# State products of a linear-attention kernel: one product of 64 value columns for each head instead of two of 32

## The chip, the cores and the metric

The kernel runs on one core of a Trainium2 chip. The metric is the device time of one execution in microseconds (us). A core has a matrix engine (TensorE, "PE" in the profile, its weight loads "PEld"), three elementwise engines (VectorE "DVE", ScalarE "ACT", GpSimd "POOL") and a queue that starts DMAs (SyncE "SP"). They run their own instruction lists in order and meet at semaphores.

## The reference, cut to what matters

Three stages follow one another: a linear attention with a decaying state, a dense layer pair (384 to 2048 and back, with an ELU between), and a routed layer pair with 8 experts. The change touches the first. It has 2 batches, 8 heads, 768 tokens and 48 features per head:

```python
for t in range(S):
    cur = np.einsum('bhd,bhe->bhde', u[None] * kt, vt)
    y[:, :, t] = np.einsum('bhd,bhde->bhe', rt, state + cur)
    state = w[None, :, :, None] * state + np.einsum('bhd,bhe->bhde', kt, vt)
...
x = moe(x)     # 1536 x 384 -> 2048 -> 384
return moe2(x) # 8 experts, 384 -> 1024 -> 384, capacity 384
```

## The kernel before

The 1536 tokens are cut into 12 chunks of 128, six for each batch. A chunk `c` costs TensorE three pieces of work: `scores(c)` (keys times queries), `outer(c)` (the sum over the chunk's tokens of key times value, which is what the chunk adds to the state), and `back(c)` (old state times queries plus masked scores times values, which is the chunk's output). The last chunk of a batch has no successor, so `outer` runs for ten chunks.

`outer(c)` multiplies `nat`, an SBUF tile that holds for each token r, the keys padded to 64 columns for each head, and the values. Keys of one head (128 tokens x 64) are the weights; values are streamed. The eight heads go as four pairs `hp` with `j` 0 and 1: head `j` writes to partitions `64*j` to `64*j+63` of the PSUM bank `u_bank(c)`, so the two heads of a pair use two column halves of the matrix engine, each with all 128 rows. The 48 value columns of a head are taken as `MAIN` = 32 columns and then 32 more that hold the remaining `REM` = 16 and 16 of zeros (`v_cols`). So there are 4 x 2 x 2 = 16 products of 64 weight columns and 32 streamed columns. All operands are float32, and each such product shows in the trace as two weight loads and two matmul records: 32 of each for a chunk. After the last, semaphore `s_u` lets DVE form the new state (`state`, L904 and L906), which `back` of the next chunk reads.

All PE work of the first two stages is one list, written out by hand. It starts with `scores(0)`, `scores(1)`, `back(0)`, `outer(0)`, `back(1)`, `outer(1)`. Then a loop runs over 6 blocks `n` of 256 tokens and 16 column tiles `f` of the dense layer. Each step issues `fc1(n, f)` (L1193 to L1195 with `xt` as the moving operand), then whatever attention piece has its slot there (`base_slot`, `step_of`), then `fc2` of three steps before (L1193 to L1195 with `g_hi`, `g_lo`). Between fc1 and fc2, DVE, ACT, DVE, ACT and POOL turn one tile into `g_hi` and `g_lo` (L1027, L726, L1030, L728, L596). fc1 waits for L1030 of two steps before. In block 0, ACT and DVE also split the weights into high and low parts as they arrive (L922 for the first layer, L928 for the second), and fc1 waits for L922 at each second `f`. POOL scales the keys by the decay in place (`natural_k1`, L523) before `outer` reads them, and prepares the rest of each chunk (L541, L547, L511, L518, L552) between its L596 steps. DVE's L886 waits for POOL's L518. Chunks 6, 8 and 10 have `outer` right behind `scores`.

Of the kernel before, what the change touches and what calls it, by code (L numbers as in the profile page):

```python
# [12 lines left out]
def build(nc, B, H, S, D, DFF, NE, FE, CAP, rkt_in, nat_in, decay, bonus, win, wout, wgate, wexp, out, slots):  # L13
    T = B * S
    C = 128
    HP = H // 2
# [20 lines left out]
    MAIN = 32  # L37
    REM = D - MAIN
    RN, KN, VM = 0, DM, DM + 64 * H
    VR = VM + MAIN * H  # L40
    NAT = VR + 3 * REM * HP
    WCH = 4
    NWC = FT // WCH
    WCOL = WCH * KT * 128
# [21 lines left out]
    def put(name, shape, dtype, at=None):  # L66

        size = int(np.prod(shape[1:])) * 4
        if at is None:
            at = top[0]  # L70
            top[0] = at + -(-size // 32) * 32
        return nc.alloc_sbuf_tensor_at(name, shape, dtype, offset=at), at + -(-size // 32) * 32

    def new(name, shape, dtype=F32):
        return put(name, shape, dtype)[0]
# [55 lines left out]

    top[0] = a_at
    rkt = [new(f"rkt{p}", [128, 2, HP, C]) for p in range(2)]
    nat = [new(f"nat{p}", [128, NAT]) for p in range(2)]
    r1 = [new(f"r1_{p}", [128, HP, C]) for p in range(2)]
    k1 = [new(f"k1_{p}", [128, HP, C]) for p in range(2)]
    att = [new(f"att_{p}", [128, 2, HP, C]) for p in range(2)]
# [17 lines left out]
    with ctx:  # L155
# [13 lines left out]
        def pair(name):  # L169
            return [sem(f"{name}{p}") for p in range(2)]  # L170
# [15 lines left out]
        s_nat = pair("nat_loaded")  # L186
# [106 lines left out]
        def chunk_at(n, f, k):  # L293

            for c in range(2, NSTEP):
                if base_slot(c) + k == FT * n + f:
                    return c
            return None
# [5 lines left out]
        def is_at(n, f, what, after=0):  # L304

            for c in range(2, NSTEP):
                if base_slot(c) + step_of(c)[what] + after == FT * n + f:
                    return c
            return None
# [9 lines left out]
        def u_bank(c):  # L319
            return ps_x2[c][:, 0:2 * C] if c < 2 else ps_u  # L320
# [19 lines left out]
        def wait_if(eng, s, count):  # L340

            if not (isinstance(count, int) and count <= 0):
                eng.wait_ge(s, count)
# [20 lines left out]
        def _(sp):  # L364
# [5 lines left out]
            def load_nat(c):  # L370
                wait_if(sp, s_rku, c - 1)
                wait_if(sp, s_y, c - 1)
                if c in (2, 3):
                    sp.wait_ge(s_u, c - 1)
                sp.dma_start(nat[c % 2][:, :], nat_in[c, :, :]).then_inc(s_nat[c % 2], 16)

            def load_nat_rk(c):
                sp.dma_start(nat[c][:, 0:VM], nat_in[c, :, 0:VM]).then_inc(s_nrk[c], 16)
# [1 line left out]
            def load_nat_v(c):  # L380
                sp.dma_start(nat[c][:, VM:NAT], nat_in[c, :, VM:NAT]).then_inc(s_nat[c], 16)

# [25 lines left out]
            load_rkt(2)  # L408
            load_out(0)
            load_nat(2)  # L410
            load_in(2)
            load_in(3)
            load_out(1)
            load_rkt(3)
            load_out(2)
            load_nat(3)
            load_out(3)
            sp.dma_start(gate_w[:, :, :], wgate).then_inc(s_gw, 16)
            sp.wait_ge(s_const, NPOOLC)
            for c in range(4, NSTEP):  # L420
                load_rkt(c)
                load_nat(c)
                if c - 4 < NBLANK // 2:
                    blank_rows(c - 4)
# [763 lines left out]
        def _(pe):  # L1188
            mm = nc.tensor.matmul

            def product(dst, w_hi, w_lo, x_hi, x_lo, start, stop):

                mm(dst, w_hi, x_hi, start=start, stop=False)  # L1193
                mm(dst, w_hi, x_lo, start=False, stop=False)  # L1194
                return mm(dst, w_lo, x_hi, start=False, stop=stop)  # L1195
# [17 lines left out]

            def v_cols(c, hp, j):

                h = 2 * hp + j
                main = VM + MAIN * h
                rem = VR + 3 * REM * hp + REM * j
                return nat[c % 2][:, main:main + MAIN], nat[c % 2][:, rem:rem + MAIN]

            def outer(c):

                pe.wait_ge(s_k1n, c + 1)
                if c < 2:
                    pe.wait_ge(s_nat[c], 16)
                else:
                    pe.wait_ge(s_xhi, 2 * c)
                    pe.wait_ge(s_xlo, 2 * c)
                for hp in range(HP):
                    for part in range(2):  # L1230
                        for j in range(2):
                            key_cols = slice(KN + 128 * hp + 64 * j, KN + 128 * hp + 64 * j + 64)
                            at = 64 * hp + MAIN * part
                            last = mm(u_bank(c)[64 * j:64 * j + 64, at:at + MAIN], nat[c % 2][:, key_cols],  # L1234
                                      v_cols(c, hp, j)[part], start=True, stop=True, skip_group_check=True)
                last.then_inc(s_u, 1)

            def back(c):
# [28 lines left out]
                for j in range(2):  # L1267
                    for hp in range(HP):
                        mm(dst(2 * j, hp), v_cols(c, hp, j)[0], att[p][:, j, hp, :], start=not old, stop=True,
                           skip_group_check=True)  # L1270
                for j in range(2):
                    for hp in range(HP):
                        last = mm(dst(1, hp), v_cols(c, hp, j)[1], att[p][:, j, hp, :], start=False, stop=j == 1,
                                  skip_group_check=True)
# [7 lines left out]
            for hp in range(HP):  # L1282
                last = nc.tensor.transpose(ps_y[1][:, 128 * hp:128 * hp + 128], pwk2[:, hp, :], ident[:, :])
# [4 lines left out]
            scores(1)  # L1288
            back(0)
            outer(0)  # L1290
            back(1)
            outer(1)

            def fc1(n, f):
# [69 lines left out]
            for n in range(NB):  # L1364
                for f in range(FT):
                    fc1(n, f)
                    c = chunk_at(n, f, 0)
                    if c is not None:
                        scores(c)
                    c = is_at(n, f, OUTER)  # L1370
                    if c is not None and leaves_state(c):
                        outer(c)
                    c = is_at(n, f, BACK)
                    if c is not None:
                        back(c)
                    if n and f == F_T:
                        for t in range(BT):
                            x2_transpose(n - 1, t)
                    if n and f == F_LG:
                        logits(n - 1)  # L1380
                    if n and f == F_CNT:
                        count(n - 1)
                    if n == NB - 1 and f == F_A:
                        early_x()
                    if f >= LAG:
                        fc2(n, f - LAG)
                    elif n:
                        fc2(n - 1, FT + f - LAG)
# [16 lines left out]
            def tile_fc2(f):  # L1405
                g = slice(f * C, (f + 1) * C)
                cols = slice(W1 + f * DM, W1 + (f + 1) * DM)
                return product(ps_y[0][:, 0:DM], ge_hi_tile[:, g], ge_lo_tile[:, g], we_hi[:, cols],
                               we_lo[:, cols], f == 0, f == ET - 1)
# [26 lines left out]
            for f in range(ET // 2, ET):  # L1436
                last = tile_fc2(f)
# [79 lines left out]
            for kt in range(KT):  # L1517
                last = nc.tensor.transpose(ps_xt[0][:, 128 * kt:128 * kt + 128], xrow[0][:, 1, 128 * kt:128 * kt + 128],
                                           ident[:, :])
# [7 lines left out]
            for kt in range(KT):  # L1527
                last = mm(ps_e[0][:, :], xe_lo[0][:, kt, C:SN], we_hi[:, kt * FE:kt * FE + HALF], start=False,
                          stop=kt == KT - 1)
# [7 lines left out]
            for f in range(ET):  # L1537
                if f % (ET // 2) == 0:
                    pe.wait_ge(s_gelo, ET // 2 + f)
                last = tile_fc2(f)  # L1540
# [9 lines left out]
            with pe.If(over > SN):  # L1550
                with pe.Fori(0, NOVER) as e:
                    pe.wait_ge(s_dld, 32 * (e + 1))
                    for kt in range(KT):
                        last = nc.tensor.transpose(ps_xt[0][:, 128 * kt:128 * kt + 128],
                                                   xrow[0][:, 0, 128 * kt:128 * kt + 128], ident[:, :])
# [3 lines left out]
                    for f in range(ET):  # L1559
                        for kt in range(KT):  # L1560
                            cols = slice(kt * FE + f * 128, kt * FE + (f + 1) * 128)
                            last = product(ps_e[f % 2][:, 0:128], we_hi[:, cols], we_lo[:, cols],
                                           xe_hi[0][:, kt, 0:128], xe_lo[0][:, kt, 0:128], kt == 0, kt == KT - 1)
# [3 lines left out]
                        last = product(ps_ye[0][:, 0:DM], ge_hi[:, f % 4, 0:128], ge_lo[:, f % 4, 0:128],  # L1567
                                       we_hi[:, cols], we_lo[:, cols], f == 0, f == ET - 1)
# [73 lines left out]
```

## Time and profile before

| | |
|---|---|
| Time, median of 3 runs | 444.85 us (444.45 to 445.5) |
| Profiled execution, its own time | 444.44 us |
| Its span, first to last instruction | 442.7 us |
| PE busy | 424.6 us (96%) |
| DVE, ACT, POOL busy | 246.0, 183.3, 232.2 us |
| Mean granted TensorE clock | 0.996 |
| Attention and dense layers | from 0 to about 284 us |
| Routed layers | from about 284 us to the end |

Busy time is the union of an engine's instructions, and a matmul's recorded duration covers more than the time for which it holds the engine. So what a group of products costs is read from its first start to the start of what comes next on PE, not from its durations.

### The profile page before, as it was taken

To read this page: it belongs to the slowest core of one execution; us is meant where nothing else is said; L and a number is where in the kernel's file an instruction comes from. 1 tells how busy PE (TensorE), PEld (TensorE's weight loads), DVE (VectorE), ACT (ScalarE), POOL (GpSimd) and SP (SyncE) were. 2 spreads that over 40 slices of the span, in tenths; PEclk is the share of its full clock that TensorE was granted. 3 is DMA by queue.
4 is the path that set the end of the run, shared out by engine and by line. 5 is a ranking of instruction groups with operands and counts; after the bars stand their busy time and mean duration, and the time that the engine had idled before them with its cause. 6 is when DMAs were issued, how large, how long until landed. Compare 5 with 4: busy or idle time off the path is not lost.

```text
span 442.7 us, 9569 instructions
## 1 busy us (share of the span) xinstructions
PE 424.6 (96%) x3764; PEld 406.0 (92%) x3764; DVE 246.0 (56%) x595; ACT 183.3 (41%) x390; POOL 232.2 (52%) x240
## 2 busy tenths in 40 slices
PE   8789999999999999999999999989999999999994
PEld 7679999999999999899999999876999999999994
DVE  7978763665366536744564477553355454553521
ACT  4256542333332323243333445333454564465520
POOL 1888775549554955396534334114434726628431
PEclk9999999999999999999999999989999999999999
DMA  7993977113200311020008000720837548357100
GB/s 248 391 402 114 377 243 281 56 40 108 80 33 23 125 48 66 3 99 2 1 14 327 0 1 36 286 89 13 291 91 304 207 147 339 131 215 299 54 31 26
DMA packets 16826, 62.40 MB, mean 141 GB/s; under 512 B 2043, under 2 KB 9509, under 8 KB 14736
## 3 DMA queue, kind: packets, MB, share of 16 engines
q1 hardware_dynamic: 14992, 57.08, 35.8%
q0 software_dynamic: 1792, 4.73, 2.8%
q8 instruction: 29, 0.48, 0.4%
q14 instruction: 13, 0.11, 0.1%
HBM read 49.38 MB, written 13.21 MB: 141 GB/s over the span
## 4 chain that ended last, share of the span: by engine, by line
PE 70%; POOL 11%; issue 7%; DVE 7%; DMA 2%; ACT 2%; SPq 0%; POOLq 0%; DVEq 0%; ACTq 0%
PE bank L1193 20%; PE bank L1195 19%; PE bank L1194 19%; POOL g_lo L596 3%; DMA rkt<-rkt 2%; PE bank L1351 2%; PE bank L1234 1%; POOL slots L574 1%; POOL nat L523 1%; ACT elu L726 1%; DVE elu L1027 1%; PE bank L1338 1%; POOL rku L511 1%; DVE elu L1030 1%; POOL rku L518 1%
## 5 line engine op out<-in xcount | busy, mean ns | idle before, releaser
L596 POOL TENSOR_TENSOR g_lo<-elu,g_hi 128x256 fp32r<-128x256 f32 x95 | 74.7, 786 | 102.6 <-ACT g_hi L728 101.3
L726 ACT ACTIVATE elu<-elu 128x256 f32<-128x256 f32 x96 | 40.2, 418 | 111.3 <-DVE elu L1027 111.2
L1193 PE MATMUL bank<-xt,wd_hi 128*128 128x256 f32 x288 | 81.6, 284 | 2.5 <-DVE wd_lo L922 1.2
L1195 PE MATMUL bank<-xt,wd_lo 128*128 128x256 f32 x288 | 81.1, 281 | 0.0
L1194 PE MATMUL bank<-xt,wd_hi 128*128 128x256 f32 x288 | 81.0, 281 | 0.0
L1027 DVE TENSOR_SCALAR elu<-bank 128x256 f32<-128x256 f32 x96 | 40.3, 420 | 49.9 <-PE bank L1195 49.6
L1193 PE MATMUL bank<-wd_hi,g_hi 128*128 128x384 f32 x192 | 67.4, 351 | 0.0
L1030 DVE SCALAR_TENSOR_TENSOR elu<-elu,bank 128x256 f32<-128x256 f32 x96 | 40.4, 421 | 47.9 <-ACT elu L726 47.4
L1194 PE MATMUL bank<-wd_lo,g_hi 128*128 128x384 f32 x192 | 64.5, 336 | 0.0
L1195 PE MATMUL bank<-wd_hi,g_lo 128*128 128x384 f32 x192 | 64.4, 336 | 0.0
L728 ACT CAST g_hi<-elu 128x256 fp32r<-128x256 f32 x96 | 39.0, 406 | 46.8 <-DVE elu L1030 45.8
L1193 PEld LDWEIGHTS bank<-xt,wd_hi 128*128 128x128 f32 x288 | 54.1, 188 | 4.2 <-DVE elu L1030 2.2
L1195 PEld LDWEIGHTS bank<-xt,wd_lo 128*128 128x128 f32 x288 | 54.5, 189 | 0.0
L1194 PEld LDWEIGHTS bank<-xt,wd_hi 128*128 128x128 f32 x288 | 54.3, 189 | 0.0
L1128 DVE SCALAR_TENSOR_TENSOR ge_lo<-bank,ge_hi 128x256 fp32r<-128x256 f32 x56 | 23.8, 425 | 49.2 <-ACT ge_hi L783 49.2
L611 POOL TENSOR_TENSOR wd_lo<-wd_raw,wd_hi 128x1024 fp32r<-128x1024 f32 x12 | 28.5, 2396 | 37.2 <-ACT wd_hi L796 24.2
L783 ACT ACTIVATE ge_hi<-bank 128x256 fp32r<-128x256 f32 x56 | 21.5, 385 | 54.2 <-PE bank L1195 26.9
L1193 PEld LDWEIGHTS bank<-wd_hi,g_hi 128*128 128x128 f32 x192 | 36.4, 189 | 1.7 <-issue 1.0
L1194 PEld LDWEIGHTS bank<-wd_lo,g_hi 128*128 128x128 f32 x192 | 36.4, 190 | 0.0
L1195 PEld LDWEIGHTS bank<-wd_hi,g_lo 128*128 128x128 f32 x192 | 36.0, 188 | 0.0
L611 POOL TENSOR_TENSOR we_lo<-we_raw,we_hi 128x1024 fp32r<-128x1024 f32 x9 | 21.3, 2398 | 26.9 <-ACT we_hi L796 26.9
L1193 PE MATMUL bank<-we_hi,ge_hi 128*128 128x384 f32 x64 | 22.5, 351 | 2.2 <-DVE ge_lo L1083 2.2
(199 smaller groups left out, 964.3 us busy)
## 6 DMA issues: line engine op xcount, KB each, us to landing
we_raw<-wexp SPq DMA_DIRECT2D x8, 1536.0 KB, 7.5
wd_raw<-wexp SPq DMA_DIRECT2D x8, 1536.0 KB, 7.6
nat<-nat SPq DMA_DIRECT2D x10, 672.0 KB, 4.3
rkt<-rkt SPq DMA_DIRECT2D x12, 512.0 KB, 6.5
xrow<-slots SPq DMA_DIRECT2D x16, 193.0 KB, 7.1
wd_raw<-win SPq DMA_DIRECT2D x4, 768.0 KB, 8.7
wd_raw<-wout SPq DMA_DIRECT2D x4, 768.0 KB, 10.5
slots<-blank SPq DMA_DIRECT2D x1, 2702.0 KB, 14.0
```

What stands on the lines that cost most here:

```text
L596: nc.gpsimd.tensor_tensor(g_lo[:, f % 4, :], elu[:, f % 2, :], g_hi[:, f % 4, :].bitcast(F32), ALU.subtract).then_inc(s_glo, 1)
L611: nc.gpsimd.tensor_tensor(EL[r][:, cols], ER[r][:, cols], EH[r][:, cols].bitcast(F32), ALU.subtract).then_inc(s_elo2[r], 1)
L726: nc.scalar.activation(elu[:, f % 2, :], elu[:, f % 2, :], ACT.Exp).then_inc(s_exp, 1)
L728: nc.scalar.copy(g_hi[:, f % 4, :], elu[:, f % 2, :]).then_inc(s_ghi, 1)
L783: nc.scalar.activation(ge_hi[:, f % 4, :], ps_e[f % 2][:, 0:SN], ACT.Relu).then_inc(s_gehi, 1)
L1027: V.tensor_scalar_min(elu[:, f % 2, :], ps_h[f % 2][:, 0:BN], 0.0).then_inc(s_m, 1)
L1030: V.scalar_tensor_tensor(out=elu[:, f % 2, :], in0=elu[:, f % 2, :], scalar=-1.0, in1=ps_h[f % 2][:, 0:BN], op0=ALU.add, op1=ALU.max).then ...
L1128: V.scalar_tensor_tensor(out=ge_lo[:, f % 4, :], in0=ps_e[f % 2][:, 0:SN], scalar=0.0, in1=ge_hi[:, f % 4, :].bitcast(F32), op0=ALU.max, o ...
L1193: mm(dst, w_hi, x_hi, start=start, stop=False)
L1194: mm(dst, w_hi, x_lo, start=False, stop=False)
L1195: return mm(dst, w_lo, x_hi, start=False, stop=stop)
L1351: last = mm(ps_lg[:, NE * t:NE * (t + 1)], x2t[:, t, 128 * kt:128 * kt + 128], gate_w[:, kt, :], start=kt == 0, stop=kt == KT - 1)
```

## The change

The values of a pair of heads are laid out differently in `nat`: main columns of head 1, main columns of head 0, remainder of head 0, 16 zeros, remainder of head 1 (112 columns for a pair, as many as before). Head 0's 64 columns then lie in one run, and head 1's are two runs of 32 whose starts lie 80 columns apart. `outer` streams them as one moving operand of 2 x 32 columns, written to the same 64 PSUM columns as before. Its 16 products of 32 columns become 8 of 64. The SBUF tile `nat` is 48 columns wider (the second run's view reaches past the data), so tiles behind it move by 192 or 384 bytes; the bytes that a DMA brings are the same. `back` takes its two 32-column pieces from their new places. The host lays out the input.

```diff
-    VR = VM + MAIN * H
-    NAT = VR + 3 * REM * HP
+    VP = 2 * MAIN + 3 * REM
+    NAT = VM + VP * HP
...
-    nat = [new(f"nat{p}", [128, NAT]) for p in range(2)]
+    nat = [new(f"nat{p}", [128, NAT + 3 * REM]) for p in range(2)]
...
-                h = 2 * hp + j
-                main = VM + MAIN * h
-                rem = VR + 3 * REM * hp + REM * j
+                main = VM + VP * hp + MAIN * (1 - j)
+                rem = VM + VP * hp + 2 * MAIN + REM * j
                 return nat[c % 2][:, main:main + MAIN], nat[c % 2][:, rem:rem + MAIN]
+
+            def v_both(c, hp, j):
+
+                step = MAIN + 3 * REM if j else MAIN
+                main = VM + VP * hp + MAIN * (1 - j)
+                return nat[c % 2][:, main:main + 2 * step].rearrange("s (k n) -> s k n", k=2)[:, :, 0:MAIN]
...
                 for hp in range(HP):
-                    for part in range(2):
-                        for j in range(2):
-                            key_cols = slice(KN + 128 * hp + 64 * j, KN + 128 * hp + 64 * j + 64)
-                            at = 64 * hp + MAIN * part
-                            last = mm(u_bank(c)[64 * j:64 * j + 64, at:at + MAIN], nat[c % 2][:, key_cols],
-                                      v_cols(c, hp, j)[part], start=True, stop=True, skip_group_check=True)
+                    for j in range(2):
+                        key_cols = slice(KN + 128 * hp + 64 * j, KN + 128 * hp + 64 * j + 64)
+                        last = mm(u_bank(c)[64 * j:64 * j + 64, 64 * hp:64 * hp + 64].rearrange("p (k n) -> p k n", k=2),
+                                  nat[c % 2][:, key_cols], v_both(c, hp, j), start=True, stop=True,
+                                  skip_group_check=True)
                 last.then_inc(s_u, 1)
```

Nothing changes places in any engine's list. On PE, the rows from `back(0)` to the first fc1 stood like this before (numbers behind `x` count equal rows; 64x32 is partitions and columns of the result):

```order
 L1269 MATMUL bank<-att_104,nat_98 32x128 x8
 L1273 MATMUL bank<-att_104,nat_98 32x128 x8
 L1234 MATMUL bank<-nat_98 64x32 x16
 L1262 MATMUL bank<-r_1_101,z_110 32x128 x8
 L1265 MATMUL bank<-r_1_101,z_110 32x128 x4
```

and stand like this now (L1234 is L1237, and the lines of `back` are four higher):

```order
 L1273 MATMUL bank<-att_104,nat_98 32x128 x8
 L1277 MATMUL bank<-att_104,nat_98 32x128 x8
 L1237 MATMUL bank<-nat_98 64x64 x8
 L1266 MATMUL bank<-r_1_101,z_110 32x128 x8
 L1269 MATMUL bank<-r_1_101,z_110 32x128 x4
```

The other nine places read alike: 16 products of 32 columns became 8 of 64. DVE, ACT, POOL and SP have the same lists as before.

## Rows read from the trace of the kernel before

**Rows 1.** The page: busy time, and shares of the chain that ended last.

```profile
PE 424.6 (96%) x3764; PEld 406.0 (92%) x3764; DVE 246.0 (56%) x595; ACT 183.3 (41%) x390; POOL 232.2 (52%) x240
...
PE 70%; POOL 11%; issue 7%; DVE 7%; DMA 2%; ACT 2%; SPq 0%; POOLq 0%; DVEq 0%; ACTq 0%
```

**Rows 2.** L1234 alone by stretch: length, PE and PEld busy (count), clock, DMA.

```profile
0.00:29.20 29.20, 2.44 (x64) 2.11 (x64) 1.00 0.90 338
29.20:53.10 23.90, 2.25 (x64) 2.03 (x64) 1.00 0.74 258
53.10:245.00 191.90, 6.75 (x192) 6.08 (x192) 1.00 0.27 94
```

**Rows 3.** PE in order, 63.9 to 68.5 us: start, length, engine, work.

```profile
63.92 1.16 PE L1209 MATMUL bank<-r,k 64*128 64x128 f32 x16
65.01 0.44 PE L1193 MATMUL bank<-wd_hi,g_hi 128*128 128x384 f32 x1
...
67.34 1.12 PE L1234 MATMUL bank<-nat 128*64 128x32 f32 x32
68.40 0.44 PE L1193 MATMUL bank<-wd_hi,g_hi 128*128 128x384 f32 x1
```

**Rows 4.** PE in windows of 0.02 to 0.3 us: same columns, length to the last end.

```profile
67.34 0.25 PE L1234 MATMUL bank<-nat 128*64 128x32 f32 x2
...
67.34 0.31 PE L1234 MATMUL bank<-nat 128*64 128x32 f32 x4
...
67.34 0.37 PE L1234 MATMUL bank<-nat 128*64 128x32 f32 x6
...
63.92 0.49 PE L1209 MATMUL bank<-r,k 64*128 64x128 f32 x4
...
63.92 0.83 PE L1209 MATMUL bank<-r,k 64*128 64x128 f32 x10
```

**Rows 5.** PE in order, part of `back` of one chunk, 73.4 to 74.4 us.

```profile
73.44 0.62 PE L1269 MATMUL bank<-att,nat 128*32 128x128 f32 x16
73.87 0.62 PE L1273 MATMUL bank<-att,nat 128*32 128x128 f32 x16
```

**Rows 6.** POOL, DVE, PE in order, 17 to 30 us; [idle before <-what ended it].

```profile
17.10 1.28 POOL L541 TENSOR_TENSOR k<-rkt,pwk 128x512 f32<-128x512 f32 x1 [1.11 <-issue]
...
23.68 0.55 DVE L886 TENSOR_REDUCE bon<-rku 128x8 f32<-128x384 f32 x1 [0.48 <-POOL rku L518]
...
27.60 1.50 DVE L922 TENSOR_TENSOR wd_lo<-wd_raw,wd_hi 128x768 fp32r<-128x768 f32 x1
...
29.24 0.36 PE L1193 MATMUL bank<-xt,wd_hi 128*128 128x256 f32 x1 [1.24 <-DVE wd_lo L922]
```

**Rows 7.** DVE and PE, 33 to 54 us; last, DVE's waits for PE, 24 to 59.

```profile
33.60 0.95 DVE L922 TENSOR_TENSOR wd_lo<-wd_raw,wd_hi 128x768 fp32r<-128x768 f32 x1
...
51.70 0.95 DVE L928 TENSOR_TENSOR wd_lo<-wd_raw,wd_hi 128x768 fp32r<-128x768 f32 x1
53.09 0.42 DVE L1027 TENSOR_SCALAR elu<-bank 128x256 f32<-128x256 f32 x1 [0.44 <-PE bank L1195]
...
34.79 0.28 PE L1193 MATMUL bank<-xt,wd_hi 128*128 128x256 f32 x1
...
DVE elu L1027 <- PE bank L1195: 0.4, 1, 0.4
```

**Rows 8.** PEld's waits, 100 to 200 us (total, times, longest), then POOL, DVE in order.

```profile
PEld bank L1234 <- POOL nat L523: 0.7, 3, 0.2
...
107.93 1.27 POOL L523 TENSOR_TENSOR nat<-nat,pwn 128x512 f32<-128x512 f32 x1
...
112.74 0.42 DVE L1027 TENSOR_SCALAR elu<-bank 128x256 f32<-128x256 f32 x1 [2.61 <-PE bank L1195]
...
135.69 0.43 DVE L1027 TENSOR_SCALAR elu<-bank 128x256 f32<-128x256 f32 x1 [0.94 <-PE bank L1195]
```

**Rows 9.** All engines, 270 to 300 us; the number behind POOL's count is the clock.

```profile
270.00:300.00 30.00, 27.73 (x158) 24.56 (x157) 18.27 (x49) 12.85 (x24) 7.65 (x9) 0.94 0.41 152
```

More of the change, by code:

```diff
@@ L374, in load_nat @@
                     sp.wait_ge(s_u, c - 1)
-                sp.dma_start(nat[c % 2][:, :], nat_in[c, :, :]).then_inc(s_nat[c % 2], 16)
+                sp.dma_start(nat[c % 2][:, 0:NAT], nat_in[c, :, :]).then_inc(s_nat[c % 2], 16)
             def load_nat_rk(c):
@@ L1599, in natural @@
         k_pad[:, :, :, :D] = k
-        rem = np.zeros((n, c, HP, 3, REM), np.float32)
-        rem[:, :, :, 0] = v[:, :, 0::2, MAIN:]
-        rem[:, :, :, 2] = v[:, :, 1::2, MAIN:]
-        return np.concatenate([r.reshape(n, c, -1), k_pad.reshape(n, c, -1), v[:, :, :, :MAIN].reshape(n, c, -1),
-                               rem.reshape(n, c, -1)], axis=2)
+        v_pair = np.zeros((n, c, HP, 2 * MAIN + 3 * REM), np.float32)
+        v_pair[:, :, :, 0:MAIN] = v[:, :, 1::2, :MAIN]
+        v_pair[:, :, :, MAIN:2 * MAIN + REM] = v[:, :, 0::2]
+        v_pair[:, :, :, 2 * MAIN + 2 * REM:] = v[:, :, 1::2, MAIN:]
+        return np.concatenate([r.reshape(n, c, -1), k_pad.reshape(n, c, -1), v_pair.reshape(n, c, -1)], axis=2)
     def per_head(a):
```

## The prediction, made before the changed kernel ran

> **What bounds the kernel now.** I read the page first. PE is busy 96% of the span and holds 70% of the chain that ended last [rows 1], so time taken off PE counts unless PE then waits for something else. The second view is the edited line by stretch [rows 2]: its 320 records are 32 for each of ten chunks, two chunks before 29.2 us, two more up to 53.1, six after. The third is PE in order of time, which tells what one call of `outer` costs: it starts at 67.34 and the next fc2 starts at 68.40, so 1.06 us [rows 3]. Ten of them are 10.6 us, 2.4% of the span. Last come the waits around these places [rows 6 to 8], because the three kinds of place differ.
>
> **What sets the 1.06 us.** The windows that cut into one `outer` show records in pairs, one for each column half. From the second pair to the third the last end moves from 0.31 to 0.37 us, and over the whole group from 0.25 (first pair) to 1.12 (sixteenth): 0.87/15 = 0.058 us a pair [rows 3, 4]. The next work starts 0.06 us before the last recorded end (68.46 against 68.40). Is that pace set by the weight loads (64 columns) or by streaming 32 columns? `scores` has twice the weight columns (128) and four times the streamed ones (128), also two tiles at a time. It moves from 0.49 to 0.83 us over three pairs, 0.11 us each [rows 4], about twice the pace of `outer`, not four times. And `back` streams 128 columns with only 32 weight columns in four tiles: 16 records in 73.87 - 73.44 = 0.43 us, 0.11 us for each record of a tile [rows 5]. So 0.11 is the price of streaming 128 columns, 64 would cost 0.055 and 32 would cost 0.027. `outer` pays 0.058 where its stream needs 0.027: the loads set its pace, one 64-column load for each half in 0.058 us. With 64 streamed columns the stream takes 0.055 and stays under the load.
>
> **The sum for one `outer`.** Removed: 16 of 32 load-and-product records. Added: 32 more columns in each remaining one. After it there are 8 pairs at 0.058. The first pair ends 0.25 us after the start with 32 columns; with 128 it ends at 0.49 - 0.11 = 0.38 [rows 4]; between them for 64 columns, 0.29. The group then takes 0.29 + 7 x 0.058 = 0.70 us to its last end, and the next work starts 0.065 earlier, at 0.63 (the same difference is 0.07 in `scores`, 65.08 against 65.01 [rows 3]). Saved: 1.06 - 0.63 = 0.43 us. Bounds: the best is half of `scores`, 1.09/2 = 0.55, so 0.51 us saved. The worst without overlap of load and stream is 0.29 + 7 x 0.11 - 0.065 = 1.0, so 0.06 saved. A streamed operand in two runs has no row in this trace. If a break costs nothing, the 0.43 stands; if it made each column cost four times as much, a pair would take 0.22, the whole 1.77 and the change would lose 0.71. I take 0.43, because it is nearest to both measured paces.
>
> A rule speaks against this. The Trainium skill, "TensorE: Matmul & The Clock Gate", section "What overlaps and what doesn't", says that a weight load overlaps running products only where its row group differs; both halves here use all 128 rows. By it load and stream add up: 0.11 us a pair after the change, and nothing is won. But it would also make the pair before 0.058 + 0.027 = 0.085, and the trace has 0.058; in `back`, whose tiles also span all rows, 32-column loads add nothing to the 0.11 us of the stream. The trace disagrees with the rule, so I use the row and keep the rule as a rival.
>
> **Which of the ten count.**
> The first two, at 15 and 19 us: none. DVE's L886 at 23.68 waits for POOL's L518, and POOL's own list had stood still 1.11 us before L541 at 17.10 for something that PE does not give (the row says issue; I take it for the arrival of `rkt`). From there DVE goes on to L922, which ends at 29.10 and releases PE at 29.24 after 1.24 us of idle time [rows 6]. PE reaching that wait 0.86 us earlier only waits longer. Bound: 0 to 0.86 us.
> The third and fourth, at 30.5 and 49.6: together 0.44. fc1 of tile 6 starts at 34.79, its weights' L922 ends at 33.60 + 0.95 = 34.55; the least distance seen is 29.24 - 29.10 = 0.14. So only 0.24 - 0.14 = 0.10 of the third's 0.43 passes. From 24 to 59 us DVE waits for PE once, 0.44 us at 53.09; its L928 ends at 52.65 [rows 7]. PE would offer 0.10 + 0.43 = 0.53 by then, DVE can use 0.44. `back` of chunk 3 waits for the state that DVE makes behind it. Bound: 0 to 0.86.
> The last six, from 67 to 200 us: 6 x 0.43 = 2.58. Three (109.25 and its two likes) wait for POOL's L523, 0.2 us or so each [rows 8]. That is a wait in front of `outer`, so the saving behind it passes; and the POOL and DVE work that leads to it is itself started by PE: DVE stands idle 2.61 us before 112.74 and 0.94 us before 135.69, each ended by PE's fc1 [rows 8]. All this moves with PE, as 0.94 is more than 0.43.
> Behind 200 us there are no more such products. What follows is started by PE's own progress and moves as a block.
>
> **The rest costs nothing.** The DMA of `nat` brings the same bytes. `back` reads pieces of the same size from other columns. SBUF tiles move by at most 384 bytes; no row shows a price for an address, and I give it none (bounds: 0.1 us either way). The state's PSUM columns stay, so DVE's reads do.
>
> **Sum.** 0 + 0.44 + 2.58 = 3.0 us. The profiled execution took 444.44 us, so 441.4; it lay 0.41 under the median 444.85 of the runs, from which it would be 441.8. I predict 441.6. A measurement here tells some 0.2% (0.9 us) from no change.
>
> **Rivals.**
> Half overlap: load and half of the stream add up, 0.058 + 0.027 = 0.085 a pair, 0.29 + 7 x 0.085 - 0.065 = 0.82, 0.24 saved; (6 + 1) x 0.24 = 1.7, time 442.9. For it: in `outer` the pace is 0.058, a little over the 0.055 which half of `scores` would give, so something small is not hidden. Against it: `back`.
> No overlap, by the rule above: 0.06 x 7 = 0.4 saved, 444.2. Against it: the pace before.
> POOL takes over: L523 in front of `outer` at 109, 154 and 199 us keeps its absolute time. Then only the product behind the last of these waits counts, 0.43 us: 444.2. For it: POOL is what PE waits for there, three times. Against it: POOL's chain starts from waits that PE ends, as above.
> All ten count, if the start is led by PE after all: 10 x 0.43 = 4.3, 440.3. Against it: the 1.24 us of idle PE at 29.24.
> Slower: the streamed operand of head 1 jumps 80 columns in the middle, and a stream in two runs is read at a quarter of the rate. Pace 0.22, 0.71 us lost in each: the eight that PE leads lose 5.7 us, and the first two some of their 1.4 where they eat the wait: 450. It decides from a pair over 0.12 us, where 0.29 + 7 x 0.12 - 0.065 = 1.06. For it: no such operand in this trace. Against it: only one jump in 64 columns, and only in half of the products.
> The clock is a disturbance more than a rival: the granted clock falls to 0.94 over 270 to 300 us, behind an idle PE [rows 9]. That is 0.06 x 30 = 1.8 us at one level of loss; that PE work comes 3 us earlier could move or drop that stretch, so plus or minus 1 us is in my range.
>
> **Chances.** Forecast 0.73 (its own range 440.6 to 442.8), all ten 0.05, half overlap 0.07, no overlap 0.07, POOL 0.04, slower 0.04. Faster by over 0.2%: 0.73 + 0.05 + 0.07, less 0.02 for the clock, 0.83. Within 0.2%: 0.07 + 0.04 + 0.02 = 0.13. Slower: 0.04. The range that leaves out at most two in ten goes from 440.3, all ten, to 443.5, past half overlap.
>
> **What would show it.** In the profile after, an `outer` has 16 records, the next PE work starts 0.63 us after its start, and a pair takes 0.058. PE's idle time before 29.2 us grows by up to 0.86 us, most of it at the wait for L922, which ends at the same time. fc1 of tile 6 waits about 0.3 us for L922. DVE's idle time before its L1027 at about 52.7 is gone. The products behind `scores` of chunks 6, 8 and 10 start 0.87, 1.73 and 2.59 us earlier (0.44 and one, three and five times 0.43), the first of them at 108.4. A pair at 0.085 or more, or a start of PE after the first wait earlier than 28.8, makes my sum wrong at its first or its second step.

## The result, and the profile after

The changed kernel takes 441.21 us (median of 7 runs, 440.71 to 442.81) against 444.41 for the kernel before on the same chip (443.96 to 445.5). The ratio is 0.9935, 95% interval 0.9917 to 0.9953, so 2.9 us less, between 2.1 and 3.7. Its profiled execution took 441.02 us with a span of 439.3. The forecast was 3.0 us, and the time forecast was 441.6.

The edited line in the changed kernel, by stretch as in [rows 2], has half the records (the first row has 32 for two chunks) and 6.86 us of busy time instead of 11.44:

```profile
0.00:29.20 29.20, 1.37 (x32) 1.09 (x32) 1.00 0.89 343
29.20:53.10 23.90, 1.37 (x32) 1.09 (x32) 1.00 0.70 243
53.10:245.00 191.90, 4.11 (x96) 3.28 (x96) 1.00 0.28 95
```

PE in order at chunk 4, as in [rows 3], then windows that end in the first, second and third pair of records, as in [rows 4]:

```profile
67.71 0.69 PE L1237 MATMUL bank<-nat 128*64 128x64 f32 x16
68.33 0.44 PE L1193 MATMUL bank<-wd_hi,g_hi 128*128 128x384 f32 x1
...
67.71 0.28 PE L1237 MATMUL bank<-nat 128*64 128x64 f32 x2
...
67.71 0.34 PE L1237 MATMUL bank<-nat 128*64 128x64 f32 x4
...
67.71 0.39 PE L1237 MATMUL bank<-nat 128*64 128x64 f32 x6
```

One `outer` now holds PE for 68.33 - 67.71 = 0.62 us instead of 1.06. The pace is (0.69 - 0.28)/7 = 0.058 us a pair, that of before with twice the streamed columns. This is the first step of the prediction, and it holds.

The start of the program does not. POOL, DVE and PE in order in the changed kernel, as in [rows 6]:

```profile
17.25 1.93 POOL L541 TENSOR_TENSOR k<-rkt,pwk 128x512 f32<-128x512 f32 x1 [1.10 <-issue]
19.14 0.61 POOL L552 TENSOR_TENSOR zw<-z,w_end 128x256 f32<-128x256 f32 x1
19.72 1.90 POOL L547 TENSOR_TENSOR r<-rkt,pw 128x512 f32<-128x512 f32 x1
22.04 1.01 POOL L511 TENSOR_TENSOR rku<-nat 128x384 f32<-128x384 f32 x1 [0.43 <-DMA nat<-nat]
23.20 1.01 POOL L518 TENSOR_TENSOR rku<-rku,u_nat 128x384 f32<-128x384 f32 x1
...
17.10 0.95 DVE L922 TENSOR_TENSOR wd_lo<-wd_raw,wd_hi 128x768 fp32r<-128x768 f32 x1
...
29.70 0.36 PE L1193 MATMUL bank<-xt,wd_hi 128*128 128x256 f32 x1 [1.24 <-DVE wd_lo L922]
```

fc1 of tile 4 starts at 29.70, 0.46 us later than before, though fc1 of tile 0 starts 0.42 us earlier (19.63 against 20.05). Of the 0.46, 0.15 come from L541, which starts that much later in this execution. L541 takes 1.93 us where it took 1.28 [rows 6]. POOL then waits 0.43 us for chunk 2's `nat`. In the kernel before, the same four instructions behind L541 read:

```profile
18.34 1.33 POOL L552 TENSOR_TENSOR zw<-z,w_end 128x256 f32<-128x256 f32 x1
19.64 1.18 POOL L547 TENSOR_TENSOR r<-rkt,pw 128x512 f32<-128x512 f32 x1
20.79 1.72 POOL L511 TENSOR_TENSOR rku<-nat 128x384 f32<-128x384 f32 x1
22.65 1.00 POOL L518 TENSOR_TENSOR rku<-rku,u_nat 128x384 f32<-128x384 f32 x1
```

DVE and POOL around 54 us, as in [rows 7]:

```profile
52.15 0.95 DVE L928 TENSOR_TENSOR wd_lo<-wd_raw,wd_hi 128x768 fp32r<-128x768 f32 x1
53.10 0.42 DVE L1027 TENSOR_SCALAR elu<-bank 128x256 f32<-128x256 f32 x1
54.01 0.42 DVE L1030 SCALAR_TENSOR_TENSOR elu<-elu,bank 128x256 f32<-128x256 f32 x1 [0.49 <-ACT elu L726]
54.35 1.32 DVE L922 TENSOR_TENSOR wd_lo<-wd_raw,wd_hi 128x768 fp32r<-128x768 f32 x1
...
53.67 1.19 POOL L547 TENSOR_TENSOR r<-rkt,pw 128x512 f32<-128x512 f32 x1
```

DVE's 0.44 us of idle time before L1027 is gone, as forecast. But the L922 behind it now runs beside POOL's L547 and takes 1.32 us instead of the 0.95 that this line takes elsewhere, so the state for `back` of chunk 3 gains almost nothing.

From chunk 4 on each `outer` brings what was forecast. The three waits for POOL's L523 are still there and small (as in [rows 8]), and DVE's L1027 is still released by PE, with 2.18 us of idle time instead of 2.61:

```profile
PEld bank L1237 <- POOL nat L523: 0.8, 3, 0.3
...
112.26 0.42 DVE L1027 TENSOR_SCALAR elu<-bank 128x256 f32<-128x256 f32 x1 [2.18 <-PE bank L1195]
```

The last dense tile's fc1 starts at 274.93 us against 277.11 before, 2.18 earlier. The span is 3.4 us shorter. The other 1.2 is the clock, as the first experiment shows: the view of all engines over 270 to 300 us, as in [rows 9], has the clock granted in full here.

```profile
270.00:300.00 30.00, 27.48 (x157) 23.18 (x155) 18.25 (x52) 11.55 (x23) 6.71 (x8) 1.00 0.41 152
```

### The profile page after: what moved, and what is told of

It is laid out like the page before. It is cut to its first block, busy times and chain, and to the rows that moved or that the text cites. A ratio compares the mean times of both kernels' runs of the same rounds, so it can differ in the third digit from the quotient of the medians.

```text
span 439.3 us, 9249 instructions
## 1 busy us (share of the span) xinstructions
PE 418.8 (95%) x3604; PEld 399.6 (91%) x3604; DVE 244.7 (56%) x595; ACT 183.2 (42%) x390; POOL 232.5 (53%) x240
## 4 chain that ended last, share of the span: by engine, by line
PE 65%; DVE 11%; POOL 9%; issue 8%; ACT 3%; DMA 3%; SPq 0%; POOLq 0%; DVEq 0%; ACTq 0%
PE bank L1193 18%; PE bank L1195 18%; PE bank L1194 17%; POOL g_lo L596 3%; ACT elu L726 2%; DVE elu L1027 2%; PE bank L1355 2%; DVE wd_lo L922 2%; DMA rkt<-rkt 1%; POOL slots L574 1%; DVE wd_lo L928 1%; DMA nat<-nat 1%; DVE elu L1030 1%; PE bank L1342 1%; POOL rku L518 1%
## 5 line engine op out<-in xcount | busy, mean ns | idle before, releaser
L1027 DVE TENSOR_SCALAR elu<-bank 128x256 f32<-128x256 f32 x96 | 40.3, 420 | 47.0 <-PE bank L1195 46.6
L616 POOL DMA_INDIRECT out<-yrow,tok_i x16 | 15.7, 983 | 16.6 <-DVE yrow L1148 12.2
```

Of the source, the lines that this page charges most:

```text
L616: nc.gpsimd.indirect_dma_start(out=out, out_offset=bass.IndirectOffsetOnAxis(ap=tok_i[r][:, t, :], axis=0), in_=yrow[r][:, t, :], in_offse ...
L1027: V.tensor_scalar_min(elu[:, f % 2, :], ps_h[f % 2][:, 0:BN], 0.0).then_inc(s_m, 1)
```

## The experiments

Each ratio is to the kernel before, timed beside it. The changed kernel, timed a second time, has 0.9944 (0.9924 to 0.9963). Since a time can't tell 0.4 us, the profiles are read against POOL's first L541, which starts at 16.85 to 17.64 us by run and which PE does not lead. The table holds what the profiles gave, in us behind L541; `nat` is the landing of the last packet of chunk 2's `nat`, in us of the span.

| kernel | L541 takes | `nat` | L518 | fc1 tile 4 | fc1 tile 18 | fc1 tile 95 |
|---|---|---|---|---|---|---|
| before | 1.28 | 20.72 | 5.55 | 12.14 | 52.44 | 260.01 |
| before, again | 1.28 | 20.83 | 5.55 | 12.15 | 52.46 | 260.07 |
| changed | 1.93 | 21.98 | 5.94 | 12.44 | 52.22 | 257.68 |
| changed, again | 1.93 | 22.39 | 6.09 | 12.60 | 52.41 | 257.90 |
| not first two | 1.28 | 21.11 | 5.55 | 12.14 | 51.92 | 257.35 |
| not chunk 0 | 1.29 | 21.24 | 5.54 | 12.15 | 51.92 | 257.35 |
| chunk 0, `rkt` first | 1.28 | 21.34 | 5.54 | 12.13 | 51.91 | 257.36 |
| each twice | 1.28 | 20.99 | 5.54 | 12.33 | 52.71 | 260.47 |
| 96 columns | 2.08 | 21.98 | 6.17 | 12.67 | 52.60 | 258.82 |
| bonus later | 1.94 | 22.25 | 6.19 | 11.44 | 51.74 | 257.21 |

**The kernel before, again.** No edit.

> The kernel before, once more, for a second profile. Theory (the start is set by POOL and the arrival of tiles, and a run moves it by a tenth or two): fc1 of tile 4 starts at 29.0 to 29.5 us, each outer takes 1.06 us, and the time lies within 0.2% of the kernel before. Rival (the start varies by half a microsecond from run to run anyway): fc1 of tile 4 starts 0.4 us or more away from 29.24. The stretch at half clock near 292 us may be missing here; if so the routed layers end about 1.4 us earlier.

444.17 us, ratio 1.0 (0.9983 to 1.0017). The start repeats to 0.01 us once it is counted from L541. No stretch at a lower clock lay near 292 us here:

```profile
270.00:300.00 30.00, 27.54 (x161) 24.02 (x162) 19.57 (x55) 12.74 (x23) 7.65 (x9) 1.00 0.42 152
```

From fc1 of tile 95 to the first warming product (L1442) the first profile has 298.74 - 277.11 = 21.63 us, this one 20.26, the changed kernel 20.22. So the lower clock cost 1.4 us in one execution, and it comes and goes with one and the same kernel. It is no part of the change.

**Each product twice**, to test whether the load sets the pace:

```diff
                 for hp in range(HP):
-                    for j in range(2):
+                    for _ in range(2):
+                        for j in range(2):
```

> New layout, each product of 64 columns is issued twice (the second writes the same values over the first), so there are 16 products a chunk as before, but of 64 columns. Theory (the weight load sets the pace and the stream of 64 columns hides under it): a pair of records still takes 0.058 us, an outer about 1.08 us, time equal to before within 0.5 us. Rival (load and stream add up, in part or whole): a pair takes 0.085 or 0.11 us, an outer 1.5 to 1.9 us, the ten add 3 to 8 us and the time is 447 or more.

444.58 us, ratio 1.0004 (0.999 to 1.0018). PE in order in this kernel:

```profile
67.39 1.15 PE L1238 MATMUL bank<-nat 128*64 128x64 f32 x32
68.47 0.44 PE L1193 MATMUL bank<-wd_hi,g_hi 128*128 128x384 f32 x1
```

Twice the streamed columns of the kernel before, with as many loads, cost 1.08 us against 1.06. The 32 extra columns of each product are all but free, and partial and full addition of load and stream are out.

A rival stays: a fixed cost of each load and product, whatever the columns. The kernel before has a row that speaks against it, with 128 weight columns and only 8 streamed ones:

```profile
81.50 1.40 PE L1351 MATMUL bank<-gate_w,x2t 128*128 128x8 f32 x12
82.75 0.42 PE L1193 MATMUL bank<-wd_hi,g_hi 128*128 128x384 f32 x1
```

Its 12 records take 82.75 - 81.50 = 1.25 us, 0.10 each, where 64 weight columns take 0.058 in each half. The cost grows with the weight columns, so it is the load that the change saves. No run changed the weight columns of `outer` itself.

**96 columns in three runs**, for the first three pairs of heads:

```diff
-                return nat[...][:, main:main + 2 * step].rearrange("s (k n) -> s k n", k=2)[:, :, 0:MAIN]
+                runs = 3 if hp < HP - 1 else 2
+                return nat[...][:, main:main + runs * step].rearrange("s (k n) -> s k n", k=runs)[:, :, 0:MAIN]
```

> As the changed kernel, but the first three pairs of heads of a chunk stream 96 columns in three runs instead of 64 in two; the last 32 land in columns that the next product overwrites, the fourth pair streams 64. Theory (pace is the larger of load, 0.055, and stream, 0.11/128 a column, and breaks in the stream cost nothing): the middle pairs take 0.080 to 0.085 us, an outer about 0.75 us instead of 0.615, the eight that PE leads cost 1.1 us more than the change, time 1.9 under before. Rival 1 (load and stream add up from here): 0.11 to 0.14 a pair, an outer 0.9 or more, 2.3 us or more over the change. Rival 2 (a break costs): the pace lies above 0.09.

442.18 us, ratio 0.9951 (0.9934 to 0.9968). PE's windows that end in the second, third and fourth pair, then the whole:

```profile
67.72 0.39 PE L1239 MATMUL bank<-nat 128*64 128x96 f32 x4
...
67.72 0.47 PE L1239 MATMUL bank<-nat 128*64 128x96 f32 x6
...
67.72 0.55 PE L1239 MATMUL bank<-nat 128*64 128x96 f32 x8
...
67.72 0.83 PE L1239 MATMUL bank<-nat 128*64 128x96 f32 x16
68.47 0.44 PE L1193 MATMUL bank<-wd_hi,g_hi 128*128 128x384 f32 x1
```

0.08 us a pair, which is 96/128 of 0.11. Past the load's 0.058 the stream sets the pace, at the price per column of an unbroken one. Head 1's streams have two breaks and head 0's have none (its step is 32 columns), and the pair goes at the stream's pace all the same. That removes the "slower" rival. An `outer` takes 0.75.

**Only the first two chunks.** `outer` keeps the form with two products of 32 columns for the others:

```diff
-                    for j in range(2):
+                    for part in range(1 if c < 2 else 2):
+                        for j in range(2):
...
+                            if c < 2:
```

> New layout, but only chunks 0 and 1 use one product of 64 columns; the other eight use two of 32. Theory A (faster outers at the start buy nothing, since POOL and DVE set the start): no gain, fc1 of tile 4 at 29.2. Theory B (they cost something: nat of chunk 2 is then in flight together with more weight transfers, lands later and DVE and POOL get in each other's way): fc1 of tile 4 at 29.5 to 29.8, time 0 to 0.5 us above before. Rival (they lead the start): 0.86 us faster.

443.96 us, ratio 0.9984 (0.9965 to 1.0002). The interval reaches from no change to 1.6 us less, so the time excludes neither the 0 of theory A nor the 0.86 of the rival. Its profile can't tell more: over 14 to 22 us the granted clock was 0.81, so its first outer was late and L541 came first. fc1 of tile 4 came 12.53 us behind L541.

```profile
14.00:22.00 8.00, 6.85 (x139) 5.50 (x138) 5.70 (x11) 2.65 (x6) 6.10 (x6) 0.81 0.90 333
```

**All but the first two** (the same edit with `c >= 2`).

> New layout, chunks 0 and 1 use two products of 32, all others one of 64. Theory A: as fast as the full change, 3.0 us under before. Theory B (the first two cost about 0.4 us in the full change): fc1 of tile 4 at 29.2 and fc1 of tile 33 about 1.0 us earlier than before instead of 0.48; time 0.4 us under the full change. Rival: 0.86 us slower than the full change, 2.1 under before.

441.13 us, ratio 0.9925 (0.9907 to 0.9943). The start is back to 12.14, and fc1 of tile 95 comes 2.66 us earlier than before, against 2.33 and 2.11 in the two profiles of the full change.

**The changed kernel, again.** No edit. I had put the late packet of its first profile down to chance.

> The changed kernel once more, for a second profile of its start. Theory (in its first profile one packet of chunk 2's nat came 1.25 us behind the other fifteen, by chance, and held POOL's L511): here L511 starts 20.8 to 21.3, L518 starts 5.5 to 5.65 us behind POOL's first L541 instead of 5.95, and fc1 of tile 4 starts 12.1 to 12.2 us behind that L541 instead of 12.45, so at 29.0 to 29.4. Rival (two short outers at the start make the transfers collide every time): 5.9 and 12.45 again. The time is 3.0 us under before either way, give or take 0.8.

441.76 us. My theory fell: L518 at 6.09 and tile 4 at 12.60, worse than the first time. The last packet landed 1.3 us behind the fifteenth again (22.39 against 21.05).

**Not chunk 0** (the same edit with `c > 0`).

> The changed kernel, but chunk 0 alone uses two products of 32 columns. Theory (it is the first outer, by letting DVE's L922 start ahead of POOL's L541, and chunk 2's nat be asked for earlier, that lengthens the start): L541 takes 1.28 us, L518 starts 5.55 us behind L541, fc1 of tile 4 starts 12.1 to 12.2 behind it, time at or up to 0.5 us under the changed kernel. Rival (the second outer does it): L518 at 5.9 to 6.2, fc1 of tile 4 at 12.4 to 12.7.

442.11 us, ratio 0.9924 (0.9892 to 0.9955). One slower outer, that of chunk 0, gives the whole of the lost start back. Chunk 1's short outer is worth nothing, as forecast: "not first two", where it is slow, has the same 257.35. POOL and DVE in order in this kernel:

```profile
17.15 1.29 POOL L541 TENSOR_TENSOR k<-rkt,pwk 128x512 f32<-128x512 f32 x1 [1.11 <-issue]
18.39 1.33 POOL L552 TENSOR_TENSOR zw<-z,w_end 128x256 f32<-128x256 f32 x1
19.69 1.17 POOL L547 TENSOR_TENSOR r<-rkt,pw 128x512 f32<-128x512 f32 x1
21.31 1.24 POOL L511 TENSOR_TENSOR rku<-nat 128x384 f32<-128x384 f32 x1 [0.45 <-DMA nat<-nat]
...
17.43 1.82 DVE L922 TENSOR_TENSOR wd_lo<-wd_raw,wd_hi 128x768 fp32r<-128x768 f32 x1
```

Here L541 starts 0.28 us ahead of L922 and takes 1.29 us, while L922 takes 1.82. In the changed kernel L922 starts 0.15 ahead, takes 0.95, and L541 takes 1.93. Whichever starts first runs at its own pace and the other waits it out: L922 ends 0.81 us behind L541 here (19.25 against 18.44), L541 ends 1.13 behind L922 there (19.18 against 18.05). With chunk 0's outer short, DVE's list (L906, L913, L916, L922) starts 0.4 us earlier and wins.

**Not chunk 1** (`c != 1`).

> The changed kernel, but chunk 1 alone uses two products of 32 columns. Theory as for the run beside it: the first outer is short, so L541 takes 1.93 us, L518 starts 5.9 to 6.2 us behind it and fc1 of tile 4 12.4 to 12.7. Rival (the second outer does it): 5.55 and 12.15.

441.88 us, ratio 0.9929 (0.9899 to 0.9959). No verdict: the clock fell to 0.79 over 14 to 22 us in its profile, the first outer was slow for that reason, and L541 took 1.27. L518 came 5.54 us behind L541, yet fc1 of tile 4 only at 12.40: DVE's L928 met POOL's L531 and took 1.32 us, against 1.05 in the kernel before. "Each twice" loses its 0.2 us at tile 4 in the same place (1.24). The time can't tell either.

**Chunk 3's `rkt` asked for first**, in the changed kernel:

```diff
             load_nat(2)
+            load_rkt(3)
             load_in(2)
             load_in(3)
             load_out(1)
-            load_rkt(3)
```

> The changed kernel; SP asks for chunk 3's rkt before three weight transfers instead of behind them, so fewer bytes follow chunk 2's nat at once. Theory (two causes, each about half: the order of L922 and L541, and a last packet of chunk 2's nat that lands 1.3 us behind the rest): the last packet lands by 21.2, L541 still takes 1.93, L518 starts 5.5 to 5.6 us behind L541, fc1 of tile 4 0.3 to 0.5 us earlier than in the changed kernel. Rival (the late packet has nothing to do with what follows it): no change, 5.95 or more.

442.26 us, ratio 0.9934 (0.9909 to 0.9959). No verdict on the late packet, since the clock was 0.57 over 14 to 22 us.

**Both** (that order, and chunk 0 with products of 32).

> Chunk 0 with two products of 32 columns and chunk 3's rkt asked for first. A candidate for a version faster than the changed kernel. Theory (the two edits remove the same loss of 0.4 us): as the better of the two, 0.2 to 0.6 us under the changed kernel, near 440.8; not told apart from it by the time, but by fc1 of tile 95 at 2.5 us or more earlier than before, counted from L541. Rival: weights now land too late and fc1 of tile 4 or 8 waits for L922, slower by 0.3 or more.

441.64 us, ratio 0.9916 (0.9883 to 0.9949). As "not chunk 0" to 0.02 us in the columns counted from L541, so the order of the transfers adds nothing where chunk 0's outer is long.

**One DVE instruction moved.** In the changed kernel:

```diff
-                    if n == 0 and f == 0:
+                    if n == 0 and f == 1:
                         sum_bonus(2)
```

> The changed kernel with one DVE instruction moved: L886 for chunk 2, which waits for POOL's L518, stands behind the second dense tile's L1030 and L928 instead of before its L1027. Theory (that wait, not PE, sets the start, so the two first outers gain nothing while it stands): fc1 of tile 4 starts about 1.4 us earlier than in the changed kernel, at 27.7 to 28.3, and the time is 1.0 to 1.5 us under the changed kernel, about 440. Rival 1 (weights and transfers set the start): fc1 of tile 4 stays within 0.3 of 29.2 and nothing is won. Rival 2 (the gain is lost again before 53 us, where DVE has no slack): fc1 of tile 4 early, but fc1 of tile 18 not.

441.23 us, ratio 0.9943 (0.9918 to 0.9967). fc1 of tile 4 comes 1.0 us earlier behind L541 than in the changed kernel, so L886's wait for POOL did hold the start. But tile 18 comes only 0.5 earlier, and the time shows nothing of it: rival 2, the gain is partly lost where DVE has no slack.

**The same in the kernel before.**

> The kernel before with the same DVE instruction moved. Theory (with the wait gone the start follows PE and DVE, so the two short outers are worth something only in the other kernel): fc1 of tile 4 at 28.4 to 28.8, the time 0.6 to 0.9 us under before, and the kernel with both edits is 3.4 to 3.9 us under this one, more than the 3.0 without. Rival: the same gain in both kernels, so the difference stays 3.0.

444.79 us, ratio 1.0011 (0.9997 to 1.0025), not the gain I expected. Here POOL stood 2.09 us for the moved instruction:

```profile
26.88 1.22 POOL L531 TENSOR_SCALAR_AFFINE_SELECT att<-bon 128x512 f32<-128x512 f32 x2 [2.09 <-DVE bon L886]
```

fc1 of tile 4 came 11.62 us behind L541 instead of 12.14, but that of tile 18 at 53.03 instead of 52.44, so the gain turned into a loss.

## Why the prediction was right, point by point

**One outer: right.** Forecast 0.43 us saved at 0.058 us a pair, measured 0.44. That load and stream don't add up is shown by doubling the products at the old cost, and where the stream takes over by 96 columns. The rule of the Trainium skill ("TensorE: Matmul & The Clock Gate", "What overlaps and what doesn't") that a load overlaps running products only in another row group is not what these runs show: the halves share all 128 rows, and load and stream do overlap.

**The last six: right.** Forecast 2.58. From before chunk 4's outer to fc1 of tile 95 the lead grows from -0.37 to 2.18 us, 2.55. The waits for L523 moved with PE, so POOL didn't take over. The sign given for this was met in its steps and not in its level: the products behind `scores` of chunks 6, 8 and 10 start 0.04, 0.89 and 1.75 us earlier (109.21, 152.97, 197.74), not 0.87, 1.73 and 2.59. The 0.83 or 0.84 that is missing was lost before chunk 4 (0.15 of it is L541's later start in this execution).

**The third and fourth: mis-sized.** Forecast 0.44, measured 0.08: from tile 4 to tile 18 the changed kernel gains 40.30 - 39.78 = 0.52 us behind L541 (52.44 - 12.14 against 52.22 - 12.44), of which 0.44 are chunk 4's; "not first two" has the same 39.78. I counted that DVE could start 0.44 earlier, and it did. I took the L922 behind it at 0.95 us; beside POOL's L547 it takes 1.32 (1.31 in "not first two"), and 0.37 is gone. In both it ends 0.81 us behind L547 (55.67 against 54.86; 55.31 against 54.50), the distance at which L922 ends behind L541 in "not chunk 0", so it waits for POOL. No run moved L547 alone to test it.

**The first two: wrong in sign.** Forecast 0 with a bound of 0 to 0.86; they cost 0.3 to 0.45 us (12.44 and 12.60 against 12.14). The step that failed is the claim that PE reaching the first wait earlier only waits longer. The end of chunk 0's outer also lets SP ask for chunk 2's `nat` (0.97 us ahead of L541 in the changed kernel, 0.54 in the kernel before and in "not chunk 0") and lets DVE start ahead of POOL. "Not chunk 0" shows that the first outer does it.

Of these two, the rows put the loss on `nat`. L541 takes 0.65 us longer, but from L541 to L511 POOL is busy about as long as before (1.93 + 0.61 + 1.90 + 1.01 = 5.45 us against 1.28 + 1.33 + 1.18 + 1.72 = 5.51), as L511 no longer waits out an L922. What is new is the wait for the last packet, 0.43 and 0.56 us in the two profiles. Without it L518 would have started 5.5 us behind L541, as in the kernel before (5.55). That is arithmetic on the rows; no run parted the two, since the order of transfers, meant to do it, met a lower clock. Why the packet is late stays open: in four profiles with a short first outer at full clock it came 1.3 to 1.6 us behind the other fifteen, in seven with a long one at most 0.25.

**The sum: right by size, in spite of two errors.** Both errors made the forecast too large. The profiles give 2.33 and 2.11 us without the clock, not 3.0. The timed ratios give 2.9 (2.1 to 3.7) and 2.5 (1.6 to 3.4), which hold either, so it is partly luck that the first of them lies so near 3.0. The range held.

The version without the short first outer is 0.33 to 0.55 us ahead of the changed kernel by its profile. By time that is not shown.

## What to carry to other kernels

Float32 products with few streamed columns pay for their weight loads. Count loads and not products, and widen the stream until it costs as much as the load, here about 64 columns for 64. A saving in front of a wait for another engine isn't worth zero by default: list which instruction of which engine, and which transfer, starts earlier for it, and what that one then runs beside. Where two engines wait for each other, an edit worth 0.4 us can lose most of it to an instruction that now lands beside another.

## What was not expected of the hardware

Two elementwise instructions that overlap on DVE and POOL do not share evenly: the later one waits out the earlier. L541 (POOL) and L922 (DVE) take 1.28 and 1.82 us when POOL's starts first, 1.93 and 0.95 when DVE's does, by a lead of 0.15 us. A streamed operand in three runs of 32 columns goes at the pace of an unbroken one, 0.08 us for 96.
